# Full-height sink transposes, one copy of the transposed probabilities, and the softmax epsilon on VectorE

## The chip, the cores and the metric

The kernel is one program on one core of a Trainium2 chip. The metric is the device time of one execution in microseconds (us); the kernel before is given as the median of three runs.

## The reference

The program is a chain of three blocks: attention with sink tokens and a sliding window, a mixture of experts with two experts per token, and a dense block with a Mish activation. The change is in the attention and in the part of the router's matmul that rides on it.

```python
# q, k, v: 2 x 8 heads x 768 positions x 64; n_sink = 4, window = 128
scores = scale * np.matmul(q, k.transpose(0, 1, 3, 2))
keep = is_sink | in_window
scores = np.where(keep, scores, -1000000000.0)
scores = scores - np.max(scores, axis=-1, keepdims=True)
a = np.exp(scores)
a = a / (np.sum(a, axis=-1, keepdims=True) + 1e-09)
attn = np.matmul(a, v)
...
logits = x @ w_gate            # x is attn, heads side by side: 1536 x 512
noise_scale = np.log1p(np.exp(x @ w_noise))
noisy_logits = logits + noise_scale * noise
# top 2 of 8 experts per token, then the experts and the Mish block
```

## The kernel before

**Pairs, units, groups.** Attention takes two heads at a time, eight pairs in all. A pair has six units of 128 queries (`QT` = 6, `t` = 0 to 5); `u` counts all 48 units. A unit sees its own 128 keys, the 128 keys ahead of them, and the four sinks of each head. The loop bodies handle two units per step, called a group here; a pair has three of them. `stream_loop` writes the first two pairs out, runs pairs 2 to 5 in a loop with a register as counter, and writes the last two pairs (6 and 7) out again, with routing work for the first half of the tokens put between. Every engine has its own instruction stream, in this written order, and the streams meet in semaphores.

**One unit.** TensorE computes the scores (`scores`, L1182, three f32r passes for each head, 64 contraction rows) into PSUM. VectorE merges the own and the previous block by a mask and takes the row's extreme (`merge_step`, L848 to L860). ScalarE takes the exponential (`exp_step`, L658) into `probs`, whose columns are head 0's 128 keys, four sinks of each head, head 1's 128 keys. TensorE transposes three pieces (`turn_probs`): two of 128 columns (L1214) and the 2 x 4 sink columns (L1215, result 8 rows high). ScalarE copies the first two out of PSUM (`pT_step`, L666, 128 x 256) and then the sink rows (L668, 8 x 128). GpSimd cuts the triangles of the own and the previous block out of the copy (`cut_probs`, L543 and L546). TensorE multiplies by the values (`values`, L1229 for the blocks, L1232 for the sinks). A column of ones in the values makes the row sums; `pT_sink` is preset to 1.0 and `v_sink` holds 1e-9 in its ninth row, so that this product adds the 1e-9 of the reference too. VectorE takes the reciprocal of the sums (`norm_step`, L874) and scales into `x_sb` (L878).

**A group on TensorE**: scores of units t and t+1, values of the two units before, transposes of t and t+1. **A group on VectorE**: two merges, then for each of the two units before: reciprocal, scaling, and, in the second and third group of a pair, one piece of the rounding remainder of the next pair's q or k (`qk_remainder`, L866 and L868).

**The router's gates.** Beside the values stand 2 x 16 more columns for each head, the products of V with the gate weights, so that the multiplication by the probabilities gives each head's part of `x @ w_gate` and `x @ w_noise`. `gate_parts` computes them from `v_turn` (V transposed, loaded by DMA): two tiles of 128 positions in each of three steps (L1192), and in the last step the sinks as well (L1195, `SK` = 9 columns of weights). The three steps for the next pair stand ahead of the transposes of t = 3, 4 and 5 of each pair, the first pair's at the very start. ScalarE copies the results into `v_in` and `v_sink` (`gate_step`).

**GpSimd** also prepares the first expert's weights from unit 14 on (`first_set`, L531 and L535), between the cuts. **SP** issues the loads of the coming pair, and the stores of attention's result, in one queue; at pair 4 seven transfers of 256 KB from `ident` into `y_dram` (L448) stand in it too.

**What waits for what around the change.** `values(u)` waits for `x_ready` of unit u-2 (its PSUM bank) and for the cut and the sink copy of unit u. `turn_probs(u)` waits for the exponential of unit u and for the copy of unit u-2. In the last group TensorE's order is values of unit 44, transposes of 46, values of 45, transposes of 47, then the values of 46 and 47.

**Behind the last unit** VectorE sums the gates of the second half of the tokens (`gate_sums`, L898: first units 42 to 46, then unit 47), chooses the experts and builds the index tables; the gathers and the experts' matmuls wait for these.

## Time and profile before

| | |
|---|---|
| median of 3 runs | 805.88 us (805.21 to 806.61) |
| profiled execution | 804.93 us |
| its span, first to last instruction | 803.2 us |
| mean granted TensorE clock | 0.989 |
| TensorE matmul busy | 775.8 us (97%) |
| TensorE weight load busy | 643.2 us (80%) |
| VectorE busy | 517.0 us (64%) |
| ScalarE busy | 278.8 us (35%) |
| GpSimd busy | 304.0 us (38%) |
| first to last instruction of L1229 (values) | 12.0 to 121.3 us |
| attention, routing tables, then experts | 6 to 122, to 141, to the end |

Each row names an engine: PE is TensorE's matmuls, PEld its weight loads, DVE is VectorE, ACT ScalarE, POOL GpSimd. A row of the order in time has start, duration, engine, line, operation, result<-inputs, shape and count; rows that follow one another with the same operation are merged (x4), and their duration is then that of the whole. A matmul's end is modelled, and matmuls overlap: the distance between two starts is the time that one takes of the engine. A bracket tells how long the engine stood idle before, and what ended that.

### The profile page before, as it was taken

Reading aid. Unit: us, or ns where it says so; the run is one execution under the profiler, and the core shown is the slowest. Engines: PE = TensorE matmul, PEld = TensorE weight load, DVE = VectorE, ACT = ScalarE, POOL = GpSimd, SP = SyncE. Lnnn points to the kernel's source line nnn. Section 1 sums busy time; section 2 is a strip of 40 time slices with the busy share of each in tenths; the row PEclk is TensorE's granted clock in tenths of the full one; section 3 lists DMA queues with packets and bytes.
Section 4 is the critical chain, followed back from the end, with each engine's and each line's share of the span. In section 5 each row is a group of like instructions: output and inputs, shape, how many; then the busy total and the mean of one; then the engine's idle time right before and its main releaser. Section 6 shows DMA issues by size and latency. Waiting matters only on the chain.

```text
span 803.2 us, 13152 instructions
## 1 busy us (share of the span) xinstructions
PE 775.8 (97%) x4116; PEld 643.2 (80%) x4117; DVE 517.0 (64%) x944; ACT 278.8 (35%) x553; POOL 304.0 (38%) x307
## 2 busy tenths in 40 slices
PE   9999994999999999999999999998999999999997
PEld 6888883788888888888888888786888888888886
DVE  5686876454454454454544544558998888888776
ACT  5665652203110302003030300145555555454453
POOL 3366672929281652817337554550111010000000
PEclk9999996999999999999999999999999999999999
DMA  7689562736372451715427353120100100000001
GB/s 204 184 237 304 146 207 55 208 103 199 104 223 79 125 175 37 228 62 156 144 62 227 102 184 109 37 66 1 53 27 27 53 27 27 1 28 25 1 0 53
DMA packets 61442, 86.15 MB, mean 107 GB/s; under 512 B 30104, under 2 KB 34200, under 8 KB 61400
## 3 DMA queue, kind: packets, MB, share of 16 engines
q1 hardware_dynamic: 43400, 37.23, 15.1%
q10 hardware_dynamic: 13600, 33.96, 14.1%
q0 software_dynamic: 4400, 14.42, 6.4%
q8 instruction: 23, 0.38, 0.2%
q14 instruction: 19, 0.16, 0.1%
HBM read 69.35 MB, written 16.25 MB: 107 GB/s over the span
## 4 chain that ended last, share of the span: by engine, by line
PE 88%; DVE 5%; ACT 2%; SPq 1%; issue 1%; DMA 1%; another core or an unknown queue 1%; POOL 0%; DVEq 0%; ACTq 0%; POOLq 0%
PE bank L1321 21%; PE bank L1332 21%; PE bank L1393 15%; PE bank L1374 15%; PE bank L1229 4%; PE bank L1305 3%; PE bank L1182 2%; PE bank L1298 2%; PE bank L1192 1%; PE bank L1214 1%; PE bank L1232 1%; SPq L448 1%; PE bank L1167 1%; DMA k_in<-in_k 1%
## 5 line engine op out<-in xcount | busy, mean ns | idle before, releaser
L563 POOL TENSOR_TENSOR wgt<-stage,wgt 128x1024 f32 (+1 forms) x64 | 151.2, 2403 | 106.6 <-ACT wgt L738 106.6
L1332 PE MATMUL bank<-wgt,hT 128*128 (+1 forms) x744 | 185.7, 398 | 0.0
L1321 PE MATMUL bank<-wgt,xT 128*128 (+1 forms) x744 | 182.4, 394 | 1.5 <-DVE xT L1049 1.5
L1321 PEld LDWEIGHTS bank<-wgt,xT 128*128 128x128 f32 x744 | 137.3, 188 | 28.9 <-DVE xT L1049 1.7
L1332 PEld LDWEIGHTS bank<-wgt,hT 128*128 128x128 f32 x744 | 135.2, 188 | 25.8
L738 ACT ACTIVATE wgt<-stage 128x1024 f32 (+1 forms) x64 | 61.6, 1045 | 269.6 <-PE bank L1332 259.4
L1393 PE MATMUL bank<-wgt,gT 128*128 128x512 f32 x576 | 141.2, 395 | 4.9 <-DVE gT L1110 4.9
L1374 PE MATMUL bank<-x2T,wgt 128*128 128x512 f32 (+1 forms) x588 | 138.1, 385 | 0.9 <-DVE x2T L1087 0.9
L1393 PEld LDWEIGHTS bank<-wgt,gT 128*128 128x128 f32 x576 | 108.5, 190 | 28.6 <-DVE gT L1110 6.1
L1374 PEld LDWEIGHTS bank<-x2T,wgt 128*128 128x128 f32 x588 | 108.7, 188 | 23.0 <-POOL wgt L635 1.1
L1055 DVE TENSOR_SCALAR h<-bank 128x512 f32<-128x512 f32 x62 | 42.9, 691 | 63.9 <-PE bank L1321 61.8
L1059 DVE CAST hT<-bank 128x512 fp32r<-128x512 f32 x62 | 42.9, 692 | 58.3 <-PE bank L1305 58.3
L808 ACT ACTIVATE recd<-nume,ones 128x512 f32<-128x512 f32 x48 | 34.8, 725 | 90.8 <-DVE nume L1133 90.8
L1070 DVE COPY y_sb<-bank 128x512 f32<-128x512 f32 x31 | 21.4, 692 | 69.5 <-PE bank L1332 55.9
L609 POOL DMA_INDIRECT ya<-y_dram,y_idx x10 | 10.2, 1019 | 132.0 <-PE bank L1366 114.9
L1061 DVE TENSOR_TENSOR hT<-bank,hT 128x512 fp32r<-128x512 f32 x62 | 42.9, 692 | 2.1
L1124 DVE TENSOR_SCALAR expv<-expv 128x512 f32<-128x512 f32 x48 | 20.7, 431 | 32.4 <-ACT expv L802 32.4
L795 ACT ACTIVATE gT<-nume 128x512 fp32r<-128x512 f32 x48 | 30.3, 632 | 28.0 <-DVE nume L1101 27.7
L543 POOL TENSOR_SCALAR_AFFINE_SELECT pT_own<-pT 128x256 f32<-128x256 f32 x48 | 20.9, 436 | 48.6 <-ACT pT L666 48.1
L1305 PEld LDWEIGHTS bank<-ident,h 128*128 128x128 f32 x248 | 30.6, 140 | 9.5 <-DVE h L1055 1.6
L1305 PE MATMUL bank<-ident,h 128*128 128x128 f32 x248 | 37.3, 273 | 0.5 <-DVE h L1055 0.4
L658 ACT ACTIVATE probs<-bank,rt_nb 128x132 f32<-128x132 f32 x96 | 30.1, 366 | 21.8 <-DVE rt_nb L860 21.6
(169 smaller groups left out, 963.7 us busy)
## 6 DMA issues: line engine op xcount, KB each, us to landing
stage<-in_moe_w ACTq DMA_DIRECT2D x48, 512.0 KB, 4.3
stage<-in_moe_w SPq DMA_DIRECT2D x16, 512.0 KB, 6.7
y_dram<-y_sb SPq DMA_DIRECT2D x31, 256.0 KB, 2.4
stage<-in_moe_w_in ACTq DMA_DIRECT2D x8, 512.0 KB, 4.5
stage<-in_moe_w_out ACTq DMA_DIRECT2D x8, 512.0 KB, 3.7
v_turn<-in_v_turned SPq DMA_DIRECT2D x8, 404.5 KB, 3.7
v_in<-in_v SPq DMA_DIRECT2D x8, 390.0 KB
x_dram<-x_sb SPq DMA_DIRECT2D x16, 192.0 KB, 3.2
```

What stands on the lines that cost most here:

```text
L563: nc.gpsimd.tensor_tensor(cols(parity, 1, u * UNIT, UNIT), stage[:, u, :], cols(parity, 0, u * UNIT, UNIT).bitcast(fp32), ALU.subtract).th ...
L738: nc.scalar.activation(cols(parity, 0, u * UNIT, UNIT), stage[:, u, :], ACT.Copy).then_inc(rounded, 1)
L808: nc.scalar.activation(recd[p][:], nume[p][:], ACT.Ln, bias=ones1[:, 1:2]).then_inc(ln_ready, 1)
L1055: V.tensor_scalar(h[:, half * 512:(half + 1) * 512], bank[half][:], 0.0, None, ALU.max).then_inc(h_ready, 1)
L1059: V.tensor_copy(hT[:, 0, 4 * half:4 * half + 4], src).then_inc(hT_rounded, 1)
L1061: V.tensor_tensor(hT[:, 1, 4 * half:4 * half + 4], src, hT[:, 0, 4 * half:4 * half + 4].bitcast(fp32), ALU.subtract).then_inc(hT_ready, 1)
L1229: T.matmul(OB[b][:, to:to + WIDE], (pT_prev if back else pT_own)[t % 3][:, hd, :], v_in[par][:, t - back].rearrange("p h d -> p (h d)")[:, ...
L1305: ins = T.transpose(bank[3 + half][:, n * P:(n + 1) * P], h[:, c * P:(c + 1) * P], ident[:])
L1321: ins = T.matmul(HA[half][:], xT[:, a, c, :], cols(par, b, c * F + half * 512, 512), start=c == 0 and n == 0, stop=c == NC - 1 and n == 2)
L1332: ins = T.matmul(YB[kk % 2][:], hT[:, a, c, :], cols(par, b, NC * UNIT + c * DM, DM), start=c == 0 and n == 0, stop=c == F // P - 1 and n ...
L1374: ins = T.matmul(hid_bank(fg)[:, tok], wgt[:, 0, b, c * F2 + f * P:c * F2 + (f + 1) * P], x2T[g % 2][:, a, c, tok], start=c == 0 and n == ...
L1393: ins = T.matmul(bank[s][:], gT[fg % 2][:, a, s * P:(s + 1) * P], wgt[:, 1, b, f * DM:(f + 1) * DM], start=f == 0 and n == 0, stop=f == NF ...
```

## The change

It has three parts.

1. The sink transpose gives 128 rows instead of 8: it transposes 128 columns of `probs` from the first sink on. The gate matmul of the sinks has 128 columns of weights instead of 9 (the sinks now stand ahead of the tiles in `v_turn`, so that the rest is the first tile's). The rows behind the eighth meet zeros in `v_sink`.
2. One ScalarE copy of 128 x 384 per unit takes the place of L666 and L668. `pT` has three buffers of three pieces, and `pT_sink` and its semaphore are gone. The copy waits for the cut of unit u-3 (`wait(act, pT_cut, u - 2)`) and the values of unit u-3.
3. The row of 1e-9 is gone from `v_sink`. VectorE adds 1e-9 to the sums (`row_scales`) and takes the reciprocal, both for the two units of a group at once, ahead of the two scalings. Behind the loop, each of the last two units has its own.

```diff
-    SK = 2 * NS + 1
+    SK = 2 * NS
...
-    pT = [attn.tensor(f"pT{i}", [P, 2, P], fp32) for i in range(2)]
+    pT = [attn.tensor(f"pT{i}", [P, 3, P], fp32) for i in range(3)]
...
-    pT_sink = [attn.tensor(f"pT_sink{i}", [P, P], fp32) for i in range(3)]
...
-            for i in range(3):
-                nc.gpsimd.memset(pT_sink[i][:], 1.0)
...
                 act.wait_ge(probs_transposed, u + 1)
-                wait(act, pT_cut, u - 1)
-                nc.scalar.activation(pT[b][:], TP[b][:, 0:2 * P].rearrange("p (h q) -> p h q", h=2), ACT.Copy).then_inc(pT_ready, 1)
+                wait(act, pT_cut, u - 2)
                 wait(act, pv_ready, u - 2)
-                nc.scalar.activation(pT_sink[t % 3][0:2 * NS, :], TP[b][0:2 * NS, 2 * P:3 * P], ACT.Copy).then_inc(pT_sink_ready, 1)
+                nc.scalar.activation(pT[t % 3][:], TP[b][:, 0:3 * P].rearrange("p (h q) -> p h q", h=3), ACT.Copy).then_inc(pT_ready, 1)
...
+            def row_scales(hp, par, t, count):
+
+                u, b = QT * (2 * hp + par) + t, t % 2
+                dve.wait_ge(pv_ready, u + count)
+                sums = banks[:, 6 + b:6 + b + count].rearrange("p b (h d) -> p b h d", h=2)[:, :, :, D]
+                at = slice(2 * b, 2 * (b + count))
+                V.tensor_scalar(rt["rs"][:, at].rearrange("p (b h) -> p b h", h=2), sums, 1.0e-9, None, ALU.add).then_inc(sums_padded, count)
+                dve.wait_ge(sums_padded, u + count)
+                V.reciprocal(rt["rc"][:, at], rt["rs"][:, at]).then_inc(dve_step, count)
+
             def norm_step(hp, par, t):
                 u, b = QT * (2 * hp + par) + t, t % 2
-                dve.wait_ge(pv_ready, u + 1)
-                o = out_heads(b)
-                V.reciprocal(rt["rc"][:, 2 * b:2 * b + 2], o[:, :, D]).then_inc(dve_step, 1)
                 dve.wait_ge(dve_step, u + 1)
...
                         merge_step(hp, par, t + 1)
+                    if not (first and n == 0):
+                        row_scales(*at_unit(it, n - 2), 2)
...
             stream_loop(dve, NP // 2, body)
+            row_scales(NP // 2 - 1, 1, QT - 2, 1)
             norm_step(NP // 2 - 1, 1, QT - 2)
             gate_sums(1, 0, QT - 1)
+            row_scales(NP // 2 - 1, 1, QT - 1, 1)
             norm_step(NP // 2 - 1, 1, QT - 1)
...
-                    ins = T.matmul(to[0:SK, GATE_TILES * 2 * GL:(GATE_TILES + 2) * 2 * GL], v_turn[:, VT_SINK:VT_SINK + SK],
+                    ins = T.matmul(to[:, GATE_TILES * 2 * GL:(GATE_TILES + 2) * 2 * GL], v_turn[:, VT_SINK:VT_SINK + P],
...
-                wait(pe, pT_sink_ready, u - 1)
+                wait(pe, pT_ready, u - 1)
...
-                T.transpose(TP[b][0:2 * NS, 2 * P:3 * P], probs[b][:, P:P + 2 * NS], ident[:]).then_inc(probs_transposed, 1)
+                T.transpose(TP[b][:, 2 * P:3 * P], probs[b][:, P:2 * P], ident[:]).then_inc(probs_transposed, 1)
...
-                pe.wait_ge(pT_sink_ready, u + 1)
...
-                T.matmul(out_heads(b), pT_sink[t % 3][:], v_sink[par][:],
+                T.matmul(out_heads(b), pT[t % 3][:, 2], v_sink[par][:],
```

Which instructions stand where on VectorE moves. In the first group of pair 6, written out behind the loop, VectorE has before (`rt_nb` is the bias of the exponential, `rt_rc` the reciprocals, `rt_lgs` the summed gates of the first half of the tokens):

```order
L860 TENSOR_REDUCE rt_nb<-bank 128x2
L874 RECIPROCAL rt_rc<-bank 128x2
L878 TENSOR_TENSOR x_sb<-bank,rt_rc 128x162
L874 RECIPROCAL rt_rc<-bank 128x2
L878 TENSOR_TENSOR x_sb<-bank,rt_rc 128x162
L898 TENSOR_REDUCE rt_lgs<-x_sb 128x96
L850 COPY_PREDICATED bank<-later,bank 128x2x128
```

and with the change:

```order
L856 TENSOR_REDUCE rt_nb<-bank 128x2
L872 TENSOR_SCALAR rt_rs<-bank 128x4
L874 RECIPROCAL rt_rc<-rt_rs 128x4
L881 TENSOR_TENSOR x_sb<-bank,rt_rc 128x162 x2
L901 TENSOR_REDUCE rt_lgs<-x_sb 128x96
L846 COPY_PREDICATED bank<-later,bank 128x2x128
```

Four instructions stand between the last reduction and the gate sums in both, but the first of them now needs both units' values. The same holds in every group; in the second and third group of a pair the two scalings have one `qk_remainder` behind each, as before.

At the tail, from the last group's scalings on, VectorE has before:

```order
L874 RECIPROCAL rt_rc<-bank 128x2
L878 TENSOR_TENSOR x_sb<-bank,rt_rc 128x162
L874 RECIPROCAL rt_rc<-bank 128x2
L878 TENSOR_TENSOR x_sb<-bank,rt_rc 128x162
L931 TENSOR_TENSOR rt_c<-rt_oh 128x6x8
L932 SCALAR_TENSOR_TENSOR rt_inc<-rt_seg,rt_c 128x48
L934 TENSOR_TENSOR rt_pos<-rt_inc,rt_c 128x48
L874 RECIPROCAL rt_rc<-bank 128x2
L878 TENSOR_TENSOR x_sb<-bank,rt_rc 128x162
L898 TENSOR_REDUCE rt_lgs<-x_sb 128x80
L874 RECIPROCAL rt_rc<-bank 128x2
L878 TENSOR_TENSOR x_sb<-bank,rt_rc 128x162
```

and with the change:

```order
L872 TENSOR_SCALAR rt_rs<-bank 128x4
L874 RECIPROCAL rt_rc<-rt_rs 128x4
L881 TENSOR_TENSOR x_sb<-bank,rt_rc 128x162 x2
L934 TENSOR_TENSOR rt_c<-rt_oh 128x6x8
L935 SCALAR_TENSOR_TENSOR rt_inc<-rt_seg,rt_c 128x48
L937 TENSOR_TENSOR rt_pos<-rt_inc,rt_c 128x48
L872 TENSOR_SCALAR rt_rs<-bank 128x2
L874 RECIPROCAL rt_rc<-rt_rs 128x2
L881 TENSOR_TENSOR x_sb<-bank,rt_rc 128x162
L901 TENSOR_REDUCE rt_lgs<-x_sb 128x80
L872 TENSOR_SCALAR rt_rs<-bank 128x2
L874 RECIPROCAL rt_rc<-rt_rs 128x2
```

The scaling of unit 44 moves behind the values of unit 45, and units 46 and 47 have one instruction more each.

## Rows read from the trace of the kernel before

**Rows 1.** Busy time by stretch: a steady pair (us; columns PE, PEld, DVE, ACT, POOL)
```profile
34.30:48.00 13.70, 13.70 (x125) 12.09 (x124) 10.47 (x29) 8.92 (x32) 6.98 (x13) 1.00 0.77 229
```

**Rows 2.** Order in time, TensorE, gate step of the sinks
```profile
33.13 0.58 PE L1192 MATMUL bank<-v_turn 128*128 128x96 f32 x4
33.65 0.28 PE L1195 MATMUL bank<-v_turn 128*9 128x64 f32 x2
33.86 0.44 PE L1214 MATMUL bank<-ident,probs 128*128 128x128 f32 x2
```

**Rows 3.** Order in time, TensorE, transposes of another unit
```profile
42.27 0.38 PE L1214 MATMUL bank<-ident,probs 128*128 128x128 f32 x2
42.49 0.27 PE L1215 MATMUL bank<-ident,probs 128*8 128x128 f32 x1
```

**Rows 4.** The chain that ended last, 64 to 72 us
```profile
64.04 4.96 DMA k_in<-in_k
```

**Rows 5.** Groups by line and shape, 0 to 230 us (busy us, mean ns, idle before)
```profile
L666 ACT ACTIVATE pT<-bank 128x256 f32<-128x256 f32 x48 | 18.3, 382 | 20.1 <-PE bank L1215 19.8
...
L668 ACT ACTIVATE pT_sink<-bank 8x128 f32<-8x128 f32 x48 | 12.0, 249 | 0.0
...
L1214 PEld LDWEIGHTS bank<-ident,probs 128*128 128x128 f32 x96 | 11.6, 145 | 5.9 <-ACT probs L658 3.6 <-issue 1.2
...
L1215 PEld LDWEIGHTS bank<-ident,probs 128*8 128x8 f32 x48 | 4.2, 87 | 0.0
```

**Rows 6.** Order in time, end of a group A and start of group B
```profile
37.88 0.17 DVE L874 RECIPROCAL rt_rc<-bank 128x2 f32<-128x2 f32 x1
...
38.20 0.33 DVE L878 TENSOR_TENSOR x_sb<-bank,rt_rc 128x162 f32 x1
...
38.66 0.81 POOL L543 TENSOR_SCALAR_AFFINE_SELECT pT_own<-pT 128x256 f32<-128x256 f32 x2 [2.82 <-ACT pT L666]
...
39.26 0.43 DVE L850 COPY_PREDICATED bank<-later,bank 128x256 f32<-128x256 uint32 x1 [0.73 <-PE bank L1182]
...
39.38 0.71 PE L1229 MATMUL bank<-v_in,pT_own 128*128 128x130 f32 x4
```

**Rows 7.** Order in time, TensorE and VectorE, group C of a steady pair
```profile
45.78 0.44 PE L1232 MATMUL bank<-v_sink,pT_sink 128*128 128x162 f32 x2
...
45.65 1.27 DVE L868 SCALAR_TENSOR_TENSOR qT<-q_in,qT 128x384 fp32r<-128x384 f32 x1
...
47.38 0.56 DVE L866 TENSOR_TENSOR kT<-k_in,kT 128x396 fp32r<-128x396 f32 x1
48.73 0.52 DVE L848 COPY_PREDICATED bank<-first_cut,far 128x256 f32<-128x256 uint32 x1 [0.78 <-PE bank L1182]
```

**Rows 8.** Order in time, VectorE, group A of pair 6
```profile
95.07 0.17 DVE L874 RECIPROCAL rt_rc<-bank 128x2 f32<-128x2 f32 x1
95.27 0.33 DVE L878 TENSOR_TENSOR x_sb<-bank,rt_rc 128x162 f32<-128x162 f32 x1
95.52 1.51 DVE L898 TENSOR_REDUCE rt_lgs<-x_sb 128x96 f32<-128x768 f32 x1
```

**Rows 9.** Order in time, TensorE, last group of pair 7
```profile
116.98 0.44 PE L1214 MATMUL bank<-ident,probs 128*128 128x128 f32 x2 [0.71 <-ACT probs L658]
```

**Rows 10.** Order in time, VectorE and TensorE, last four units
```profile
118.73 0.17 DVE L874 RECIPROCAL rt_rc<-bank 128x2 f32<-128x2 f32 x1 [1.23 <-PE bank L1232]
...
120.50 0.17 DVE L874 RECIPROCAL rt_rc<-bank 128x2 f32<-128x2 f32 x1 [0.52 <-PE bank L1232]
...
121.07 1.24 DVE L898 TENSOR_REDUCE rt_lgs<-x_sb 128x80 f32<-128x640 f32 x1
122.23 0.15 DVE L874 RECIPROCAL rt_rc<-bank 128x2 f32<-128x2 f32 x1
...
122.78 0.37 DVE L898 TENSOR_REDUCE rt_lgs<-x_sb 128x16 f32<-128x128 f32 x1
...
118.98 0.68 PE L1229 MATMUL bank<-v_in,pT_own 128*128 128x130 f32 x4
```

More of the change, by code:

```diff
@@ L111, in attention_moe_mish @@
     v_sink = [attn.tensor(f"v_sink{i}", [P, 2, VW], fp32) for i in range(2)]
-    VT_GATE, VT_TILES, VT_SINK = 0, 2 * GL, 2 * GL + S
+    VT_GATE, VT_SINK, VT_TILES = 0, 2 * GL, 2 * GL + SK
     WIDE = 2 * (D + 1)
@@ L142, in attention_moe_mish @@
     rt = {}
-    for name, cols in (("nb", 4), ("rc", 4), ("seg", E * QT), ("seg_e", E * QT), ("noise", E * NT), ("lgs", GL * NT),
+    for name, cols in (("nb", 4), ("rs", 4), ("rc", 4), ("seg", E * QT), ("seg_e", E * QT), ("noise", E * NT), ("lgs", GL * NT),
                        ("enx", E * NT), ("sp", E * NT), ("lg", E * NT), ("eq", E * QT), ("cum", E * QT), ("cut", E * QT),
@@ L266, in attention_moe_mish @@
         pT_ready = sem("pT_ready")
-        pT_sink_ready = sem("pT_sink_ready")
         WEIGHTS_FROM = 14
@@ L271, in attention_moe_mish @@
         x_ready = sem("x_ready")
+        sums_padded = sem("sums_padded")
         dve_step = sem("dve_step")
@@ L542, in cut_probs @@
                 wait(pool, pv_ready, u - 2)
-                ins = nc.gpsimd.affine_select(out=pT_own[b][:], in_=pT[u % 2][:], compare_op=ALU.is_ge, fill=0.0, base=0,
+                ins = nc.gpsimd.affine_select(out=pT_own[b][:], in_=pT[b][:, 0:2], compare_op=ALU.is_ge, fill=0.0, base=0,
                                               pattern=[[0, 2], [1, P]], channel_multiplier=-1)
                 if u % QT > 0:
-                    ins = nc.gpsimd.affine_select(out=pT_prev[b][:], in_=pT[u % 2][:], compare_op=ALU.is_ge, fill=0.0, base=-1,
+                    ins = nc.gpsimd.affine_select(out=pT_prev[b][:], in_=pT[b][:, 0:2], compare_op=ALU.is_ge, fill=0.0, base=-1,
                                                   pattern=[[0, 2], [-1, P]], channel_multiplier=1)
@@ L877, in norm_step @@
                     x_sb[:, t, ds(2 * hp + par, 1)].rearrange("p a h d -> p (a h) d")
-                V.tensor_tensor(to, o, rt["rc"][:, 2 * b:2 * b + 2].unsqueeze(2).broadcast_to([P, 2, VW]),
+                V.tensor_tensor(to, out_heads(b), rt["rc"][:, 2 * b:2 * b + 2].unsqueeze(2).broadcast_to([P, 2, VW]),
                                 ALU.mult).then_inc(x_ready, 1)
@@ L1451 @@
     laid["v"] = values
-    held = _np.zeros((pairs, 2 * sinks + 1, 2, dim + 1), _np.float32)
+    held = _np.zeros((pairs, 2 * sinks, 2, dim + 1), _np.float32)
     for h in range(2):
@@ L1455 @@
         held[:, h * sinks:(h + 1) * sinks, h, dim] = 1.0
-    held[:, 2 * sinks, :, dim] = 1.0e-9
     experts = inputs["moe_noise"].shape[1]
-    turned = _np.zeros((pairs, 2, dim, seq + 2 * sinks + 1 + 4 * experts), _np.float32)
-    turned[..., 4 * experts:4 * experts + seq] = inputs["v"].reshape(pairs, 2, seq, dim).transpose(0, 1, 3, 2)
+    turned = _np.zeros((pairs, 2, dim, seq + 2 * sinks + 4 * experts), _np.float32)
+    turned[..., 4 * experts + 2 * sinks:] = inputs["v"].reshape(pairs, 2, seq, dim).transpose(0, 1, 3, 2)
     gates = [inputs[n].reshape(heads // 2, 2, dim, experts) for n in ("moe_w_gate", "moe_w_noise")]
     for h in range(2):
-        at = 4 * experts + seq + h * sinks
-        turned[:, h, :, at:at + sinks] = turned[:, h, :, 4 * experts:4 * experts + sinks]
+        at = 4 * experts + h * sinks
+        turned[:, h, :, at:at + sinks] = turned[:, h, :, 4 * experts + 2 * sinks:4 * experts + 3 * sinks]
         at = 2 * h * experts
```

## The prediction

> **What bounds the kernel now.** I began with the busy time by stretch. The change touches attention alone, the first 122 us; in a steady pair of heads there TensorE is busy for 13.70 of 13.70 us, VectorE for 10.47, so a microsecond counts only where TensorE loses or gains one [rows 1]. A steady pair is therefore a sum of TensorE's steps. Then I looked for the places where TensorE waits after all: the last two pairs, where VectorE also does the routing sums, and the tail behind the last unit, where VectorE alone goes on. Everything behind the tail starts when the tail ends, so what it loses the kernel loses.
>
> I call two units a group; a pair has three, A (units 0, 1), B (2, 3) and C (4, 5). TensorE's steps are written as distances between starts, since the ends of matmuls overlap.
>
> **1. The gate matmul of the sinks, once a pair: 0.14 us off each.** In group C, TensorE runs four gate passes at L1192, the sink gate step L1195 (two passes, 9 columns of weights), then transposes. A row's last start is its start plus its time less one matmul's 0.27. So L1192's last pass starts at 33.13 + 0.58 - 0.27 = 33.44, L1195 0.21 behind it at 33.65, the first transpose at 33.86 and the second at 33.86 + 0.44 - 0.27 = 34.03 [rows 2]. Where all weights have 128 columns two transposes stand 0.38 - 0.27 = 0.11 apart [rows 3]. The four steps (two passes of L1195, two transposes) take 0.59 now and 4 x 0.11 = 0.44 then: by the rounded starts 0.15 less; I take 0.14. [...]
>
> There are eight such steps. The first stands ahead of a transpose that waits for ScalarE anyway. The one of pair 3 is lost in a stall: SP's queue, started once by pair 3's group A, brings k_in only at 69.0 [rows 4], and pair 4 waits for that whatever came before. The one of pair 6 is lost below. Five count: **-0.70 us**.
>
> **2. The sink transposes, 48 of them: nothing.** The weight load grows from 87 ns to the 145 of the other transposes [rows 5]. The distance to a narrow one is that to a wide one already: 42.27 + 0.11 = 42.38 is the second, 42.49 the narrow third [rows 3]. The load lies under the stream; if it did not, 48 x 0.058 = 2.8 us more. [...]
>
> **3. One ScalarE copy of 384 columns for two of 256 and 8 rows x 128: nothing.** The two take 0.38 and 0.25; a copy of 384 columns takes an estimated 0.51, since 128 columns take 0.25 and 256 take 0.38 [rows 5]. GpSimd's cut waits for the first copy, so it starts 0.13 later. In a steady group the first cut of two ends at 38.66 + 0.41 = 39.07 and TensorE's values start at 39.38, after its scores [rows 6]: 0.18 is left. If that cover were gone in all 24 groups the price would be 24 x 0.13 = 3.1 us at most. Where it is thin (the last two units) part 5's wait is longer. SP's queue passes the same transfers, one row or column smaller: nothing. Three memsets fewer on GpSimd at the start: nobody waits.
>
> **4. VectorE in the loop: later, and only just covered, +0.2 us.** Add and reciprocal now serve two units, and both wait for the second unit's values. As many instructions as before; what moves is the first unit's pair, which used to lie beside the second unit's matmuls. In steady group A the second reciprocal starts at 37.88, its scaling 0.32 later, then VectorE idles 0.73 until 39.26 [rows 6]. Now the add stands at 37.88, the reciprocal at 38.20, the scalings at 38.52 and 38.77; the last ends at 39.10. That is 0.16 before the next merge. Group C has two remainders more. Its second values end at 45.78 + 0.44 = 46.22; add at 46.26, then 0.31, 0.31, 0.25 and the first remainder at 47.13, the second scaling 0.47 behind its start, the second remainder 0.25 behind that, at 47.85, and its end at 48.41, where the next merge could start at 48.73 - 0.14 = 48.59 [rows 7]. By that 0.18 is left. But the last remainder now falls beside GpSimd's first cut, and such a neighbour can cost it some tenths. I take 0.05 a pair for four pairs, **+0.20**; the bounds are 0 and, with the long case of the first rival, 1.4. In group B the same delay meets ScalarE's lead.
>
> **5. VectorE in the last two pairs and the tail: +2.0 us.** These steps are unrolled, and reciprocal, scaling, next instruction stand 0.20 and 0.25 apart [rows 8].
> - Pair 6, group A. Before, the second unit's reciprocal at 95.07 is followed by the gate sums at 95.52. Now the add is at 95.07, reciprocal 95.27, scalings 95.47 and 95.72, sums 95.97: +0.45. The sums (1.51 us) run straight into the next merge [rows 8], and TensorE has no gate step ahead of the transposes that need its result. **+0.45**. It also makes VectorE the late one in the next group C, where two more sums stand, so that pair's 0.14 is not seen.
> - Pair 7, group B. The same sequence ahead of the second choice of experts; TensorE waits 0.71 for it at 116.98 already [rows 9]. **+0.45**.
> - Between them, VectorE again late by **+0.05**, an estimate.
> - The tail. The scaling of unit 44 used to stand ahead of unit 45's values. Now it waits for them: add 118.73, reciprocal 118.94, scaling 119.13 to 119.46. Unit 46's values need that bank and start at about 119.60 instead of 118.98: +0.62. Unit 46's add stands at 120.50 + 0.62 = 121.12. Now reciprocal 121.32, scaling 121.52, sums 121.88 where they were at 121.07, and 1.16 behind their start the add of unit 47 instead of its reciprocal (122.23 before): 123.04. One more instruction of 0.20 there puts the last sums at 123.80 instead of 122.78 [rows 10]. **+1.02**.
>
> **Sum.** -0.70 + 0.20 + 0.45 + 0.05 + 0.45 + 1.02 = +1.47 us on the profiled execution's 804.93, so 806.4. That execution is 0.95 under the median of the runs, 805.88; against the median, 807.3 us. I take 0.2% (1.6 us: 804.3 to 807.5) as what can be told from no change. The forecast lies within it, close to its slow end.
>
> **Rivals.**
> - *VectorE becomes the late engine inside the loop (slower).* GpSimd prepares weights there, and a remainder of q that falls beside such an operation took 1.27 us, one of k beside none 0.56 [rows 7]. The reorder leaves group C 0.18 of its 0.78 us. If one remainder grows by half of those 0.71, the merge of the next group A is about 0.2 late; if by all, 0.5; I take 0.35. Group A has no gate matmuls to hide it. It decides as soon as VectorE's idle time before L848 is gone. In four pairs that is 1.4 us, 1.2 more than the forecast has: 808.5. For it: these overlaps are common from pair 2 on. Against: moving the remainder 1.5 us later takes it out from under the operation it met there [rows 7].
> - *The new sink gate matmul still leaves gaps.* Then the 0.70 is missing: 808.0. Against: steps of 128 columns follow one another at 0.11 [rows 3].
> - *The tail and the routing groups hide the shift* (the wait on unit 44 is met, ScalarE's lead covers the rest). Then about half of 1.97, and the 0.20, are gone: 806.1. Against: VectorE goes from sums to merge and from sums to reciprocal without idle time [rows 8, 10].
> - *Wide weight loads are not hidden (slower).* 48 x 0.058 = 2.8 us: 810.1. By the Trainium skill, "TensorE: Matmul & The Clock Gate", LDWEIGHTS, a load takes time in proportion to its columns, which speaks against the change. The trace has the longer load (87 to 145 ns) and no longer distance.
> [...]
>
> **How the numbers follow.** Forecast 0.50, VectorE late in the loop 0.20, hidden 0.13, gaps stay 0.10, wide loads 0.04, drained transposes 0.03. Time: 807.3, the forecast's. Of the forecast's 0.50 I put 0.14 over 807.5, of the gap rival 0.08. Slower: 0.14 + 0.20 + 0.08 + 0.04 = 0.46. Faster: 0.03. Same: 0.51. The range runs from 805.4 (hidden, and a cheaper tail) to 809.0 (loop rival, its price 0.5 a pair in most pairs); outside lie the wide loads, the drained transposes and what a repeated measurement can shift, under 0.2. The forecast's own range is 806.3 to 808.0.
>
> **What would show it.** In the changed profile: the sink gate step 0.11 behind the last gate pass and the transposes 0.11 apart; the third transpose 0.11 behind the second; the wide copy at about 0.51; VectorE idle for some 0.16 before the merge behind group A and up to 0.2 behind group C; the time between TensorE's steady group starts shorter by 0.14 a pair; unit 46's values late behind the scaling of unit 44, and the last gate sums 2.0 us later against the start of pair 6. Wrong it would be if steady pairs grew longer, if TensorE waited longer for probabilities in group A, or if the tail were unchanged.

## The result and the profile after

The changed kernel takes 811.77 us, the median of four runs (810.52 to 812.53), beside 806.25 for the kernel before in the same session. The ratio of the runs is 1.0068, with a 95% interval of 1.0051 to 1.0086: slower by 5.5 us. I had forecast 807.3, with a range up to 809.0, and given "slower by over 0.2%" 0.46. The profiled execution took 812.53 us, its span is 810.6 us.

The page of the changed kernel, head and busy time:
```profile
span 810.6 us, 13138 instructions
PE 778.3 (96%) x4116; PEld 647.2 (80%) x4117; DVE 520.0 (64%) x946; ACT 277.3 (34%) x505; POOL 308.4 (38%) x304
```

A steady pair by stretch (us; columns as in [rows 1]), and its groups by line and shape, 0 to 230 us, against [rows 5]:
```profile
35.60:49.22 13.62, 13.48 (x126) 12.45 (x125) 9.79 (x29) 8.68 (x26) 7.62 (x14) 1.00 0.76 225
```
```profile
L664 ACT ACTIVATE pT<-bank 128x384 f32<-128x384 f32 x48 | 23.4, 491 | 19.4 <-PE bank L1222 18.9
L540 POOL TENSOR_SCALAR_AFFINE_SELECT pT_own<-pT 128x256 f32<-128x256 f32 x48 | 22.8, 476 | 48.0 <-ACT pT L664 47.7
L543 POOL TENSOR_SCALAR_AFFINE_SELECT pT_prev<-pT 128x256 f32<-128x256 f32 x40 | 20.6, 515 | 0.0
L1222 PEld LDWEIGHTS bank<-ident,probs 128*128 128x128 f32 x48 | 6.7, 140 | 0.0
```
TensorE, 13.70 of 13.70 us busy before, now has idle time in the steady pair: 13.48 of 13.62. The wide copy takes 0.49 us (I had estimated 0.51), 0.11 more than the first of the two copies before. The weight load of the sink transposes (L1222) takes 140 ns where the narrow one took 87 [rows 5]. GpSimd's cuts did not change, yet their mean grew: that of the own tile from 436 ns to 476, that of the previous tile from 453 to 515.

TensorE's gate step, order in time, against [rows 2]:
```profile
33.81 0.58 PE L1199 MATMUL bank<-v_turn 128*128 128x96 f32 x4
...
34.56 0.58 PE L1199 MATMUL bank<-v_turn 128*128 128x96 f32 x4
34.98 0.36 PE L1202 MATMUL bank<-v_turn 128*128 128x64 f32 x2
35.18 0.39 PE L1221 MATMUL bank<-ident,probs 128*128 128x128 f32 x2
```
The sink gate step starts 34.98 - (34.56 + 0.58 - 0.27) = 0.11 us behind the last gate pass. The transposes start 0.20 behind that, and stand 0.39 - 0.27 = 0.12 apart. This is as forecast, to 0.01.

**Where the time went.** I cut the attention part at starts of TensorE's instructions: the first values matmul of units 0, 24, 30, 42 and 47, and the first matmul behind the second of the two long waits for the routing (TensorE's rows at 13.21, 68.91, 84.24, 112.91, 124.42 and 140.42 in the changed kernel). Stretch I holds four pairs (0 to 24), III two (30 to 42), IV is pair 7 up to unit 47, V the tail. Left out are units 24 to 30 and all behind the tail: the first holds a wait for a transfer, both hold stretches in which TensorE got half its clock in some of the profiled executions (last section). V has such a stretch too, in every kernel, but only behind the start of the first long wait; from the end of that wait to the end of the second all kernels take 6.67 to 6.70 us, so what differs in V lies ahead of it.

Each stretch is read from one profiled execution of each kernel. How well it repeats is seen where kernels have the same instructions in it: stretch I took 55.68 to 55.71 in the changed kernel and the four runs e5 to e8, and stretch V 13.49 to 13.51 in four kernels (before, e1, e2, e9). I take differences over 0.05 us as told apart.

| us | I | III | IV | V | sum |
|---|---|---|---|---|---|
| before | 54.86 | 28.07 | 9.45 | 13.51 | 105.89 |
| changed | 55.70 | 28.67 | 11.52 | 15.99 | 111.88 |
| difference | +0.84 | +0.60 | +2.07 | +2.48 | +5.99 |

The sum answers to the 5.5 us measured (4.1 to 6.9 by the interval). Two places carry most of it. The first, in pair 7, all engines in order of time (changed kernel):
```profile
117.65 1.26 POOL L532 TENSOR_TENSOR wgt<-stage,wgt 128x512 fp32r<-128x512 f32 x1
...
117.77 1.16 DVE L929 TENSOR_TENSOR rt_gap<-rt_m,rt_m 128x6 f32<-128x6 f32 x1
...
118.86 0.42 DVE L846 COPY_PREDICATED bank<-later,bank 128x256 f32<-128x256 uint32 x1
```
```profile
120.46 0.44 PE L1221 MATMUL bank<-ident,probs 128*128 128x128 f32 x2 [1.91 <-ACT probs L655]
...
123.15 0.49 PE L1235 MATMUL bank<-v_in,pT_own 128*128 128x130 f32 x2 [0.65 <-DVE x_sb L881]
```
L929 subtracts six columns, and takes 1.16 us; the same instruction (L926) took 0.28 at this place in the kernel before, where GpSimd's weight piece started 0.23 behind it. It ends at 118.93, GpSimd's weight piece at 118.91. The merge of unit 46 stands behind it, and TensorE waits 1.91 us for that unit's exponential instead of 0.71 [rows 9]. The second row of TensorE is unit 46's values behind unit 44's scaling, 0.65, as my part 5 had it.

The second place is the tail, VectorE and GpSimd in order of time, changed kernel:
```profile
123.25 0.35 DVE L934 TENSOR_TENSOR rt_c<-rt_oh 128x48 f32<-128x48 f32 x1
123.63 0.34 DVE L935 TENSOR_TENSOR_SCAN rt_inc<-rt_seg,rt_c 128x48 f32<-128x48 f32 x1
124.00 2.61 DVE L937 TENSOR_TENSOR rt_pos<-rt_inc,rt_c 128x48 f32<-128x48 f32 x1
126.65 0.16 DVE L872 TENSOR_SCALAR rt_rs<-bank 128x2 f32<-128x2 f32 x1
...
127.40 1.22 DVE L901 TENSOR_REDUCE rt_lgs<-x_sb 128x80 f32<-128x640 f32 x1
```
```profile
123.81 2.74 POOL L554 CAST ramps<-ramp 128x3072 f16<-128x3072 f32 x1
```
and the same in the kernel before:
```profile
119.74 0.24 DVE L934 TENSOR_TENSOR rt_pos<-rt_inc,rt_c 128x48 f32<-128x48 f32 x1
120.50 0.17 DVE L874 RECIPROCAL rt_rc<-bank 128x2 f32<-128x2 f32 x1 [0.52 <-PE bank L1232]
120.71 0.33 DVE L878 TENSOR_TENSOR x_sb<-bank,rt_rc 128x162 f32<-128x162 f32 x1
```
```profile
120.23 2.74 POOL L557 CAST ramps<-ramp 128x3072 f16<-128x3072 f32 x1
```
Before, the subtraction of positions ended 0.25 us ahead of GpSimd's cast. Now it starts 0.19 behind the cast's start and ends at 126.61, 0.06 behind the cast's end. Reciprocal, scaling and sums, which have one operand in SBUF or none, ran beside the same cast at their usual 0.17, 0.33 and 1.24 us [rows 10].

My theory A: **VectorE's instructions with two SBUF operands are kept out while GpSimd runs one that reads SBUF, and the joint wait for two units moved them there.** The rivals are B, the later copy and cut; C, VectorE late anyway and the long subtractions only covering that; D, the additions themselves.

### The profile page after: what moved, and what is told of

It reads as the page before. It is cut to its first block, busy times and chain, and to the rows that moved or that the text cites. A ratio compares the mean times of both kernels' runs of the same rounds, so it can differ in the third digit from the quotient of the medians.

```text
span 810.6 us, 13138 instructions
## 1 busy us (share of the span) xinstructions
PE 778.3 (96%) x4116; PEld 647.2 (80%) x4117; DVE 520.0 (64%) x946; ACT 277.3 (34%) x505; POOL 308.4 (38%) x304
## 4 chain that ended last, share of the span: by engine, by line
PE 87%; DVE 6%; issue 2%; ACT 2%; SPq 1%; DMA 1%; POOL 0%; DVEq 0%; ACTq 0%; POOLq 0%
PE bank L1338 21%; PE bank L1327 21%; PE bank L1399 15%; PE bank L1380 15%; PE bank L1311 3%; PE bank L1235 3%; PE bank L1304 2%; PE bank L1189 2%; PE bank L1199 1%; PE bank L1238 1%; SPq L447 1%; PE bank L1221 1%; PE bank L1174 1%; DMA k_in<-in_k 1%; PE bank L1372 0%
## 5 line engine op out<-in xcount | busy, mean ns | idle before, releaser
L540 POOL TENSOR_SCALAR_AFFINE_SELECT pT_own<-pT 128x256 f32<-128x256 f32 x48 | 22.8, 476 | 48.0 <-ACT pT L664 47.7
```

## The experiments

**The parts alone.**
```diff
 e1: kernel before with
-    T.matmul(to[0:SK, ...], v_turn[:, VT_SINK:VT_SINK + SK], ...)
+    T.matmul(to[:, ...], v_turn[:, VT_SINK:VT_SINK + P], ...)
 e2: changed kernel with
-    row_scales(...)
+    V.reciprocal(rt["rc"][...], o[:, :, D])    # in norm_step, per unit
 e3: kernel before with row_scales (one for two units)
 e4: changed kernel with
-    row_scales(*at_unit(it, n - 2), 2)
+    row_scales(*at_unit(it, n - 2 + side), 1)  # ahead of each norm_step
```


> The kernel before with the gate part alone: the sink gate matmul loads 128 columns, with the sinks laid ahead of the tiles. Nothing else is changed. My part 1 (0.14 us off each of eight gate steps, five of which count): 0.7 us faster than before, 805.2 beside a before of 805.9, which a measurement can just tell. A rival: the 0.14 is swallowed by the next wait (for the exponential of the following unit), and the time is that of before within 0.2%. In both, the first values and the tail stand as in the kernel before: none of the 5.5 us of loss.

> The change without its addition of 1e-9: VectorE takes the reciprocal of each unit's row sums straight from PSUM, unit by unit, as in the kernel before (the 1e-9 is left out of the computation). The gate step, the 128-row transposes and the one ScalarE copy stay. Theory A (VectorE's order and its collisions with GpSimd's long operations are the loss): the tail is back as before, pair 7's wait is back at about 0.7 us, and the time is within 1.5 us of before (804.5 to 807.5). Theory B (the later copy and GpSimd's cut are the loss, at each unit's values): the time stays 3 us or more above before (809 or more), and the values go on starting 147 ns behind the end of the cut.

> The kernel before with the addition on VectorE alone: one addition and one reciprocal for the two units of a group (1e-9 is then added twice). Transposes, copies and gate matmuls are those of before. Theory A: this carries all or more of the loss, 5 to 7 us above before, with unit 46's values waiting for unit 44's scaling and the position cast of the tail beside GpSimd's long cast (2.6 us instead of 0.24). Theory B: it costs about 2 us (my parts 4 and 5), 807.5 to 808.5.

> The change with addition and reciprocal unit by unit, each just ahead of its unit's scaling, instead of one pair for two units: one addition and one reciprocal more per group (0.16 and 0.18 us by the profile after), but unit 44 no longer waits for unit 45. If the joint wait is what costs (unit 46's values behind unit 44's scaling, and the tail's cast that thereby falls beside GpSimd's long cast): 3 to 5 us faster than the change, 807 to 809. If the number of VectorE instructions is what costs: 1 to 3 us slower than the change, 812.5 to 815.

| | ratio to before, 95% | I | III | IV | V | sum to before |
|---|---|---|---|---|---|---|
| changed | 1.0068, 1.0051 to 1.0086 | 55.70 | 28.67 | 11.52 | 15.99 | +5.99 |
| e1 gate part | 0.9990, 0.9973 to 1.0008 | 54.31 | 27.77 | 9.45 | 13.49 | -0.87 |
| e2 no addition | 1.0002, 0.9982 to 1.0022 | 54.77 | 27.85 | 9.66 | 13.50 | -0.11 |
| e3 addition alone | 1.0056, 1.0036 to 1.0075 | 55.14 | 28.73 | 10.40 | 15.89 | +4.27 |
| e4 unit by unit | 1.0046, 1.0028 to 1.0064 | 55.08 | 28.23 | 11.11 | 13.92 | +2.45 |

Most of the loss is in the order of VectorE: without it (e2) the change stands at before, with it alone (e3) 4.3 of the 6.0 us are there, under the 5 to 7 expected, since L934, the gap, escaped its collision there (0.28 us) while the positions did not (2.61). Theory B's 809 for e2 fell. B is not empty, though: e2 stands 0.76 us over e1 by its stretches. e4 is 3.5 us faster than the change by its stretches (I had expected 3 to 5), but only 1.8 by its ratio, and by that it cannot be told from the change. Its tail is back at 13.92, since the subtraction of positions (0.28 us) now starts 0.17 ahead of the cast; L929 still took 1.16 beside GpSimd, and TensorE waited 1.92.

e1's gain of 0.87 us is in the stretches alone; its ratio cannot be told from before.

**The two collisions taken away one by one**, each in the changed kernel:
```diff
 e5 (GpSimd), ahead of the cast of the ramps:
+    pool.wait_ge(x_ready, QT * NP - 1)
 e6 (VectorE): the score gap of both batches in one, in the tail
-    score_gap(0)                               # in pair 7
-    V.tensor_tensor(rt["gap"][:, js], ...).then_inc(gap_ready, 1)
+    V.tensor_tensor(rt["gap"][:], ...).then_inc(gap_ready, 2)
 e7: both
 e8: row_scales(..., 1) per unit in the last group of pair 7 only
```


> The change with one wait added on GpSimd: its long cast of the ramps waits for the scaling of unit 46, so it can no longer start ahead of VectorE's position subtraction. Theory A (GpSimd's cast keeps that subtraction of two SBUF operands out until it ends, 2.61 us instead of 0.24): the subtraction takes 0.24 us, the first gate sums start 2.4 us earlier, and the time is 2.4 us under the change, about 809.5 beside a before of 806.5 (ratio 1.0038 instead of 1.0068). Theory C (the tail is late because VectorE had got late before, and the stretched subtraction only covers a wait that would be there anyway): no gain, within 0.5 us of the change.

> The change with the score gap of the first batch taken out of pair 7 and computed with that of the second batch, in one subtraction in the tail (nothing reads it before). Theory A: the 1.16 us stay of this subtraction beside GpSimd's weight piece goes, TensorE's wait ahead of unit 46's transposes falls from 1.91 to 0.7 to 0.9 us, and everything behind is some 1 us earlier; how the tail's cast then falls beside the position subtraction is open, so 1 to 3.4 us under the change (ratio 1.002 to 1.0055). Theory C: the exponential of unit 46 is late for other reasons, and the wait stays over 1.5 us.

> The two edits together, on the change: both subtractions of two SBUF operands stand clear of GpSimd's long operations. Theory A: 3.3 us under the change, ratio 1.0025 to 1.003; what is left, some 2 us over before, is the later order in the loop (group A's exponentials, the cuts) and unit 46's values behind unit 44's scaling (0.65). If the ratio stays above 1.005, the collisions are not where the loss is.

> The change with addition and reciprocal unit by unit in the last group of the last pair only. Unit 46's values no longer wait 0.65 us behind unit 44's scaling, at the price of two more instructions (0.34 us) on VectorE. Theory A: whether the position subtraction falls ahead of GpSimd's cast or behind its start decides: ahead of it, 2.5 to 3 us under the change (ratio about 1.0035); behind it, within 0.7 us of the change. The wait of 1.91 us ahead of unit 46's transposes stays in both.

| | ratio to before, 95% | I | III | IV | V | sum to before |
|---|---|---|---|---|---|---|
| e5 cast held | 1.0053, 1.0030 to 1.0075 | 55.70 | 28.69 | 11.53 | 14.10 | +4.13 |
| e6 gap once | 1.0050, 1.0031 to 1.0068 | 55.71 | 28.73 | 10.61 | 16.10 | +5.26 |
| e7 both | 1.0047, 1.0032 to 1.0063 | 55.68 | 28.68 | 10.60 | 14.13 | +3.20 |
| e8 last group split | 1.0042, 1.0026 to 1.0059 | 55.70 | 28.70 | 11.09 | 13.93 | +3.53 |

VectorE and GpSimd in order of time with the cast held (e5):
```profile
123.46 0.21 DVE L938 TENSOR_TENSOR rt_pos<-rt_inc,rt_c 128x48 f32<-128x48 f32 x1
124.15 0.16 DVE L873 TENSOR_SCALAR rt_rs<-bank 128x2 f32<-128x2 f32 x1 [0.49 <-PE bank L1239]
```
```profile
125.05 2.74 POOL L555 CAST ramps<-ramp 128x3072 f16<-128x3072 f32 x1 [1.74 <-DVE x_sb L882]
```
The subtraction takes 0.21 us again, and VectorE then waits for unit 46's values, 0.49. So the stretch V gives back 1.89 and not the 2.4 I expected: 0.5 us of the time at the cast would have gone to that wait anyway. In e6 TensorE's wait falls from 1.91 to 1.00, and stretch IV by 0.91, while the tail keeps its 2.61 us beside the cast. In e7 both add up, 2.8 us by the stretches. Theory C, by which neither edit would gain over 0.5 us, does not hold for these two stretches, but it has its 0.5 us in V. In e8 the positions (0.28 us) stand 0.17 ahead of the cast again, and unit 46's values no longer wait for unit 44's scaling; L929 keeps its 1.16, and TensorE waits 1.89 for the exponential as before.

The whole times say less than I had expected of them. For e5 and e7 I had forecast ratios of 1.0038 and 1.0025 to 1.003; both came out higher, 1.0053 and 1.0047, and e7's whole interval lies over its forecast, though 1.0047 is under the 1.005 at which I would have given up theory A. All four runs lie under the change's 1.0068, but their intervals overlap with its interval. And what e7 still loses, 3.2 us by the stretches, is more than the 2 that theory A left for it.

**What is left in the loop.** Unit 20 in a steady pair, VectorE, GpSimd and the start of its values, in order of time, the changed kernel and then the kernel before:
```profile
58.03 0.41 POOL L540 TENSOR_SCALAR_AFFINE_SELECT pT_own<-pT 128x256 f32<-128x256 f32 x1 [0.24 <-ACT pT L664]
58.05 0.80 DVE L864 SCALAR_TENSOR_TENSOR qT<-q_in,qT 128x384 fp32r<-128x384 f32 x1
...
58.38 0.72 POOL L543 TENSOR_SCALAR_AFFINE_SELECT pT_prev<-pT 128x256 f32<-128x256 f32 x1
...
59.00 0.55 DVE L862 TENSOR_TENSOR kT<-k_in,kT 128x396 fp32r<-128x396 f32 x1
59.06 0.76 POOL L540 TENSOR_SCALAR_AFFINE_SELECT pT_own<-pT 128x256 f32<-128x256 f32 x1
...
59.25 0.68 PE L1235 MATMUL bank<-v_in,pT_own 128*128 128x130 f32 x4
```
```profile
54.91 1.27 POOL L535 TENSOR_TENSOR wgt<-stage,wgt 128x512 fp32r<-128x512 f32 x1
...
56.81 0.40 POOL L546 TENSOR_SCALAR_AFFINE_SELECT pT_prev<-pT 128x256 f32<-128x256 f32 x1
```
```profile
55.48 1.11 DVE L868 SCALAR_TENSOR_TENSOR qT<-q_in,qT 128x384 fp32r<-128x384 f32 x1
```
Before, the remainder of q (L868, two SBUF operands) stood ahead of unit 20's cut, beside a weight piece, and did the waiting: 1.11 us instead of 0.55, and nobody waited for it. The cut took 0.40 and ended at 57.21, 0.47 ahead of the values at 57.68. In the changed kernel the remainder stands beside the cut and has started first. Now GpSimd waits, its cuts take 0.72 and 0.76 us, and TensorE's values start 0.15 behind the end of unit 20's cut (59.10). That is how far they stand behind it where TensorE visibly waits for it (unit 2 below), so here the cut came last. At this place it costs little: TensorE has no idle time ahead of unit 20's values, and units 18 to 20 take 4.31 us instead of 4.24.

It costs more where both cuts of a unit are hit. Unit 2, changed kernel, all three engines in order of time:
```profile
16.11 0.55 DVE L864 SCALAR_TENSOR_TENSOR qT<-q_in,qT 128x384 fp32r<-128x384 f32 x1
16.19 0.74 POOL L540 TENSOR_SCALAR_AFFINE_SELECT pT_own<-pT 128x256 f32<-128x256 f32 x1 [3.43 <-ACT pT L664]
...
16.81 0.56 DVE L862 TENSOR_TENSOR kT<-k_in,kT 128x396 fp32r<-128x396 f32 x1
16.88 0.76 POOL L543 TENSOR_SCALAR_AFFINE_SELECT pT_prev<-pT 128x256 f32<-128x256 f32 x1
...
17.79 0.68 PE L1235 MATMUL bank<-v_in,pT_own 128*128 128x130 f32 x4 [0.52 <-POOL pT_prev L543]
```
Each cut starts 0.07 to 0.08 us behind a remainder, and TensorE stands idle for 0.52 us. In stretches I and III the values start within 0.16 us of the end of the cut at 1 unit of 36 in the kernel before, at 3 in e2, and at 12 in the changed kernel.

There is a third kind of victim in the loop. In the second unit of each pair VectorE masks eight columns (L850; mask and fill are both in SBUF), ahead of the extreme that the exponential needs. Pair 3, changed kernel:
```profile
50.98 1.27 POOL L532 TENSOR_TENSOR wgt<-stage,wgt 128x512 fp32r<-128x512 f32 x1
51.35 0.93 DVE L850 COPY_PREDICATED bank<-later,far 128x8 f32<-128x8 uint32 x1 [0.15 <-DVE bank L846]
```
It ends at 52.28, 0.03 behind GpSimd's weight piece. It takes 0.18 us in the first pairs, and in pairs 3 to 6 0.58, 0.32, 0.58 and 0.32 in the kernel before, but 0.93, 0.67, 0.93 and 0.67 in the changed one. TensorE's wait for pair 3's exponential behind it is 0.43 us instead of 0.21.

Between 12 and 115 us 26 of GpSimd's instructions are over 0.15 us longer than the shortest of their kind; there were 14 before, and 14 in e2. The later copy and the later remainder meet in these cuts, so I took them apart:
```diff
 e9 (no addition) and e10 (the change): two copies instead of one
-    nc.scalar.activation(pT[t % 3][:], ...3 * P...).then_inc(pT_ready, 1)
+    nc.scalar.activation(pT[t % 3][:, 0:2], ...).then_inc(pT_ready, 1)
+    nc.scalar.activation(pT[t % 3][:, 2], ...).then_inc(pT_sink_ready, 1)
+    pe.wait_ge(pT_sink_ready, u + 1)           # in values
 e11: kernel before, gate part, gap as in e6, and
 e12: e4 with two copies, gap as in e6, and
+    gate_sums(1, 0, QT - 2)                    # pair 7, n == 10
     count_rows(0)
```


> The change without its addition (1e-9 left out), and with two ScalarE copies per unit: 256 columns first, which let GpSimd's cut start, then the 128 of the sinks. Against the run without the addition alone it tells what the one wide copy costs by itself. From the first values of unit 0 to those of unit 24 (four pairs) before took 54.85 us, the gate part alone 54.31, the change without the addition 54.76. If the wide copy's 0.1 us of delay of each cut makes that 0.45: 54.3 to 54.4, and a ratio of 0.998 to 1.000. If it is the 128-row transposes or the wide weight loads: still 54.7 to 54.8, ratio 0.999 to 1.001.

> The change in full, with two ScalarE copies per unit as in the run before. If the later cut and VectorE's later order work together in the loop (either alone costs 0.3 to 0.45 us over four pairs, both cost 0.85 and hide the gate part's gain): four pairs take 54.6 to 55.0 instead of 55.70, pair 7 and the tail stay (11.5 and 16.0 us), and the time is 1 us under the change, ratio about 1.0055. If the cut's delay is not it: 55.5 to 55.8.

> A version meant to beat both: the kernel before with the gate part, the score gap of both batches in one subtraction in the tail, and four of the five tiles of the second batch's gate sums made inside pair 7, in the group of units 46 and 47. Over the gate part alone: 0.2 us in pair 7, and 0.3 us in the tail, where VectorE's 1.24 us of sums made the last reciprocal late (122.23 beside values that end at 121.9). 1.2 us under before, ratio 0.998 to 0.999; a rival is that the earlier sums stand ahead of unit 46's scaling and give it back.

> How near the addition on VectorE comes to before: the change with scales unit by unit, two copies per unit, the score gap in one subtraction in the tail, and four tiles of the gate sums inside pair 7. Theory A: nothing of VectorE's later order stays but some 0.2 us of additions on the path: four pairs 54.6 to 54.9, pair 7 at 9.6 to 10.2 instead of 11.5, the tail at 13.6 to 14.0 instead of 16.0; ratio 0.9995 to 1.0015. If the 1e-9 on VectorE costs by its instructions: ratio over 1.003.

| | ratio to before, 95% | I | III | IV | V | sum to before |
|---|---|---|---|---|---|---|
| e9 no addition, two copies | 0.9993, 0.9977 to 1.0008 | 54.36 | 27.76 | 9.45 | 13.51 | -0.81 |
| e10 change, two copies | 1.0059, 1.0041 to 1.0078 | 55.10 | 28.57 | 11.33 | 15.90 | +5.01 |
| e11 | 1.0017, 1.0003 to 1.0031 | 54.32 | 27.74 | 9.39 | 15.82 | +1.38 |
| e12 | 1.0045, 1.0027 to 1.0063 | 54.35 | 28.01 | 9.84 | 16.20 | +2.51 |

e9 stands at the gate part alone (-0.87): the 128-row transposes and their loads cost nothing, the one wide copy 0.70 us (e2 less e9). In the full change it costs 0.98 (changed less e10), 0.60 of it in stretch I. Most of that is unit 2: with the shorter copy its first cut starts ahead of the remainder and takes 0.41, only the second is hit (0.73), and TensorE does not wait. I had expected 54.6 to 55.0 in stretch I; it is 55.10. e12 shows the joint wait itself: the additions unit by unit, with two copies, leave stretch I at 54.35, where the joint addition had 55.10.

e11 and e12 were to be gains and were losses, in one stretch: V. VectorE and GpSimd in e11, in order of time:
```profile
119.06 1.03 DVE L898 TENSOR_REDUCE rt_lgs<-x_sb 128x64 f32<-128x512 f32 x1
120.01 2.81 DVE L930 TENSOR_TENSOR rt_c<-rt_oh 128x48 f32<-128x48 f32 x1
122.85 0.26 DVE L931 TENSOR_TENSOR_SCAN rt_inc<-rt_seg,rt_c 128x48 f32<-128x48 f32 x1
```
```profile
119.98 2.74 POOL L557 CAST ramps<-ramp 128x3072 f16<-128x3072 f32 x1
```
I had put the earlier sums ahead of the counts, and the addition of the counts then started 0.03 us behind the cast: 2.81 us for 48 columns. The collision of the change, made again at another instruction, in a kernel without the addition of 1e-9. In e12 the same addition (L935 there) starts 0.22 behind the cast and takes 2.62. This left open whether anything is lost without collisions, and gave a test of the explanation: the same sums behind the counts.
```diff
 e13: e12 without the earlier gate sums
 e14: e11 with
+    count_rows(0)
     gate_sums(1, 0, QT - 2)
-    count_rows(0)
```


> The change with scales unit by unit, two ScalarE copies per unit, and the score gap of both batches in one subtraction in the tail; the gate sums stay where they are. Theory A (the loss is VectorE's operations of two SBUF operands behind GpSimd's, and the later cut): four pairs 54.35 us, pair 7 at 9.8, the tail at 13.9 if the counts stand ahead of GpSimd's cast, so within 0.5 us of before in these stretches, ratio 1.000 to 1.0015. Theory D (the additions cost by being there): the tail stays over 15 us or the loop over 55, ratio over 1.003.

> The kernel before with the gate part, one score gap in the tail, and four tiles of gate sums inside pair 7, now behind the counts instead of ahead of them. Theory A: the addition of the counts no longer starts 0.03 us behind GpSimd's cast, it takes 0.35 us instead of 2.81, and the tail takes 13.3 to 13.6 us instead of 15.82; ratio 0.998 to 0.9995. If the earlier sums themselves are what costs, the tail stays over 15 us.

| | ratio to before, 95% | I | III | IV | V | sum to before |
|---|---|---|---|---|---|---|
| e13 | 1.0012, 0.9995 to 1.0030 | 54.38 | 28.01 | 9.86 | 13.97 | +0.33 |
| e14 | 0.9994, 0.9979 to 1.0008 | 54.32 | 27.75 | 9.40 | 13.24 | -1.18 |

VectorE and GpSimd in e14, in order of time:
```profile
119.03 0.24 DVE L930 TENSOR_TENSOR rt_c<-rt_oh 128x48 f32<-128x48 f32 x1
...
119.88 1.03 DVE L898 TENSOR_REDUCE rt_lgs<-x_sb 128x64 f32<-128x512 f32 x1
```
```profile
120.09 2.74 POOL L557 CAST ramps<-ramp 128x3072 f16<-128x3072 f32 x1
```
The order of two calls exchanged, and the tail is 2.58 us shorter (15.82 to 13.24). The sums, with one SBUF operand, run beside the cast at their 1.03 us. In e13 the addition of the counts (0.24 us) starts 0.85 ahead of the cast, and the tail is at 13.97. Here the whole times speak too: e14 is 1.9 us under e11 by the ratios (0.0023) and e13 2.7 under e12 (0.0033), each against before in its own session; the intervals of these differences, estimated from those of the runs, are 0.0020 and 0.0025 to either side.

e13 keeps the gate part, the 128-row transposes and the addition of 1e-9 on VectorE; what it gives up of the change is the joint addition for two units and the one wide copy, and it moves the gap. It cannot be told from before. Theory D fell. The version that is best by its stretches is e14, 1.2 us under before; by its ratio it cannot be told from before either.

## Why the prediction was wrong

| term of the sum | forecast | by the stretches |
|---|---|---|
| 1. gate step | -0.70 | -0.87 (e1) |
| 2. sink transposes | 0 | +0.06 (e9 less e1) |
| 3. one wide copy | 0 | +0.70 (e2 less e9) |
| 4., 5. VectorE in the loop, pair 6, between | +0.20, +0.45, +0.05 | +1.75 (changed less e2, I and III) |
| 5. pair 7 | +0.45, +0.62 | +1.86 (same, IV) |
| 5. tail | +0.40 | +2.49 (same, V) |

**Parts 1 and 2 were right.** The distances are those forecast, and 0.14 us a step was right: e1 gains 0.55 in I, which holds four steps, and 0.30 in III, which holds two. I had counted five, since that of pair 3 is followed by the wait in units 24 to 30, which the stretches leave out. The transposes of eight columns had no gap to give back, and widening them costs no more than 0.06. The rival that the gaps stay is out, and no run shows narrow transposes that drain, to which I gave 0.03. Wide loads do not show either: the load grew from 87 to 140 ns, which is far less than in proportion to its columns (8 and 128), and nothing waited for it.

**Part 3 failed at "0.18 is left".** That cover was read at one unit, the first of a pair, which has one cut and not two, at 0.41 us. In the kernel before the values of units 8, 44, 46 and 47 already start 0.15 us behind the end of their cut, and there nothing is left: 0.21 of the 0.70 us stand in IV. GpSimd's cuts also have a wait of their own where VectorE's remainders have started first, and then the 0.11 later copy is on the path; and a copy 0.11 later can be what puts the cut behind the remainder, as at unit 2.

**Part 4 named the right neighbours and the wrong loser.** It said that the remainder would fall beside GpSimd's cut and "can cost it some tenths". It was the cut that lost them, 0.31 and 0.35 us in the rows of unit 20, and this cost time where TensorE had to wait for the cut (0.52 us at unit 2). The rival "VectorE becomes the late engine inside the loop" had the sign, and the smaller part of the mechanism. For four pairs it had 1.4 us; the change loses 0.93 in stretch I (changed less e2). TensorE's idle time there rose from 0.50 to 1.46 us: 0.74 more ahead of values, where it waits for cuts, and 0.22 more ahead of transposes, where it waits for exponentials. The rival priced only the second. Of the 0.82 us in stretch III 0.47 are the first group of pair 6, where part 5 had 0.45; the other five groups lose 0.06 to 0.07 each.

**Part 5 was right in what it counted.** Unit 46's values wait 0.65 behind the scaling of unit 44 (forecast 0.62). With the gap moved, pair 7 loses 0.95 (e6 less e2, IV) where I had 1.07; with the cast held, the tail loses 0.60 (e5 less e2, V) where I had 0.40. **The step that failed is that I moved a sequence later on VectorE, by 0.45 us and more, and costed each instruction at its old duration.** The two that crossed the start of a GpSimd instruction grew by 0.9 and 2.4 us. Taking these collisions away gives back 2.8 us by the stretches (e7), of the 4.5 between the forecast's +1.5 and the 6.0 that the stretches show; the rest is the loop's and the wide copy's.

The rows to see it were there: in the trace of before, the subtraction of positions ends over 0.2 us ahead of a cast of 2.74 us. I looked at what waits for the shifted instructions, and not at what they would then stand beside. The Trainium skill has the rule, "SBUF — State Buffer", Who interferes with whom: a VectorE instruction with two SBUF inputs contends with a GpSimd instruction that reads SBUF, and whichever starts second is blocked for the whole of the other. The trace agrees to 0.1 us at four places, where the blocked instruction is short: 118.93 behind 118.91, 126.61 behind 126.55, 52.28 behind 52.25, and in e11 122.82 behind 122.72. A longer one ends later, the cut of unit 20 0.25 us behind the remainder (59.10 and 58.85). It also agrees on what does not contend: one SBUF operand, or PSUM as the other (the reciprocal, the scaling and the sums beside the cast).

What stays open: the ratios alone separate the change from e1, e2, e9, e11, e13 and e14; they do not separate it from e3 to e8, e10 and e12, for which the reading rests on the stretches of one profiled execution each. The 1.75 us in the loop were divided by TensorE's idle time and not by an edit for each cause; e13 less e9 shows that without the wide copy and the joint wait they are gone but for 0.3. No run takes the collisions with GpSimd's cuts away and leaves the joint wait.

## What to carry to other kernels

Where a change makes VectorE late, list its instructions with two SBUF operands behind that place and the GpSimd instructions that read SBUF around them: one that crosses a GpSimd start waits for its end, however small it is (8 columns took 0.93 us, 48 columns 2.61). Give such instructions a chosen place (ahead of the long one, or hold that one back by a wait that costs nothing), instead of leaving it to tenths of a microsecond. One instruction for two units also waits for the later unit: it saves an issue and delays the first result, here 0.75 us over four pairs (e10 less e12), although unit by unit takes more instructions.

## What the runs showed of the hardware that I had not expected

**The start decides who pays.** A remainder on VectorE paid 0.56 us beside GpSimd's weight piece in the kernel before (1.11 instead of 0.55), and made GpSimd's cut pay 0.31 in the changed one, where it had started ahead of that cut. Here it was the start that decided, and not the kind of instruction or its length.

**Half the clock, at places that move.** From within the first of its long waits for the routing on TensorE was granted 0.50 of its clock, 1.2 instead of 2.4 GHz (129.9 to 146.9 us in the changed kernel, where the wait is 126.1 to 133.7), and in some kernels again a little later. By stretch, columns as in [rows 1], first e2, which had its full clock back and fell again, then e13, which kept it at that place:
```profile
141.50:148.30 6.80, 6.05 (x14) 4.79 (x15) 1.22 (x2) 3.03 (x4) 6.77 (x4) 0.50 0.55 150
```
```profile
141.70:148.30 6.60, 5.09 (x26) 4.07 (x26) 2.08 (x3) 4.24 (x5) 5.79 (x5) 1.00 0.55 152
```
The same happened behind the wait for k_in in units 24 to 30, in e9 behind a wait of 1.90 us:
```profile
71.85 0.44 PE L1212 MATMUL bank<-ident,probs 128*128 128x128 f32 x2 [1.90 <-ACT probs L656]
```
```profile
72.30:79.10 6.80, 6.75 (x35) 6.09 (x35) 2.28 (x8) 3.33 (x12) 3.78 (x6) 0.50 0.97 316
```
but not in e13 behind one of 1.98 us at 70.86. Units 24 to 30 took 15.2 to 16.4 us at full clock and 17.6 to 19.3 with such a stretch, and all behind the tail 668.6 to 672.2, with no step in common with the edits. The whole times go with it. Executions of the kernel before lie up to 5.8 us apart (804.6 to 810.4 in 97 executions of four sessions, up to 5.6 us within one session), and their mean granted clock is 0.987 or 0.989 in all that took under 806 us, and 0.981 to 0.985 in all that took over 808. Where in those executions the clock fell is not known, since only one of each kernel was profiled. e5 was 2.4 us ahead of the changed kernel at the end of V and only 0.7 at the end. So a comparison by stretches said more here than one of whole times.
